# Routing logits of twelve token tiles: from matmuls on turned rows to products and sums on VectorE

## What is computed

```python
skip_score = x @ w_skip            # 512 numbers
do_compute = skip_score > 0
logits = xc @ w_gate               # 512 x 8
e_idx = np.argmax(logits, axis=1)
gate_w = softmax(logits)[e_idx]
out[do_compute] = xc + gate_w * (relu(xc @ w1[e]) @ w2[e])
```

## Time and profile before

| | us |
|---|---|
| median of 3 runs | 864.53 (864.14 to 866.72) |
| the profiled execution | 864.83 |
| its span, first to last instruction | 863.1 |
| attention and block 0, up to the first copy of x2 | 294.9 |
| blocks 1 to 4, told by the copies of x2 | 71.6 each |
| block 5 and the experts | 281.8 |

### The profile page before, as it was taken

How to read it: one execution, slowest core, us unless ns; L and a number is a source line. 1 busy time by engine, 2 the same in 40 slices (tenths; PEclk the granted TensorE clock), 3 DMA queues, 4 the chain that set the end, 5 groups by cost and what they waited for, 6 DMA issues and landing times.

```text
span 863.1 us, 15119 instructions
## 1 busy us (share of the span) xinstructions
PE 828.5 (96%) x4870; PEld 687.4 (80%) x4871; DVE 463.4 (54%) x1122; ACT 358.1 (41%) x870; POOL 228.9 (27%) x232
## 2 busy tenths in 40 slices
PE   5999999998799999999999999999998899999995
PEld 4777777775799998899898989989986677887884
DVE  4766676666533344435434444443665699375342
ACT  4766766674233322222232222222344387255241
POOL 3656655661444001001001001100011232222121
PEclk9999999999899999999999999999999999999998
DMA  6344444521425102021021010001142499455100
GB/s 145 96 110 120 122 117 109 156 68 54 148 62 179 73 19 92 1 83 27 3 74 28 10 73 1 25 1 74 55 129 102 146 322 343 163 173 182 31 26 8
DMA packets 97200, 80.93 MB, mean 94 GB/s; under 512 B 63420, under 2 KB 74940, under 8 KB 97152
## 3 DMA queue, kind: packets, MB, share of 16 engines
q1 hardware_dynamic: 94096, 75.31, 28.4%
q0 software_dynamic: 3056, 5.00, 1.8%
HBM read 65.18 MB, written 18.25 MB: 97 GB/s over the span
## 4 chain that ended last, share of the span: by engine, by line
PE 69%; DVE 2%; issue 1%; DVEq 1%; ACT 0%; POOL 0%; POOLq 0%; ACTq 0%
PE h_ps L1495 11%; PE out_ps L1495 11%; PE h_ps L1496 11%; PE h_ps L1497 11%; PE out_ps L1497 11%; PE out_ps L1496 11%; PE lg_ps L1546 2%; PE out_ps L1622 1%; PE tr_ps L1535 1%; PE tr_ps L1587 1%; DVEq L845 0%; DVE ht_lo L1261 0%; DVE xt_lo L1222 0%; DVE x2t L1251 0%; DVE tile_ids L1231 0%
## 5 line engine op out<-in xcount | busy, mean ns | idle before, releaser
L1352 ACT ACTIVATE ex<-h_ps 128x384 f32<-128x384 f32 x96 | 47.3, 493 | 295.5 <-PE h_ps L1497 295.5
L1191 DVE TENSOR_SCALAR ex<-ex 128x384 f32<-128x384 f32 x96 | 35.2, 366 | 229.8 <-ACT ex L1352 229.8
L1495 PE MATMUL h_ps<-xt_hi,wi_hi 128*128 128x384 f32 x384 | 134.0, 349 | 5.2 <-DVE xt_lo L1222 5.2
L1496 PE MATMUL h_ps<-xt_lo,wi_hi 128*128 128x384 f32 x384 | 130.7, 340 | 0.0
L1497 PE MATMUL h_ps<-xt_hi,wi_lo 128*128 128x384 f32 x384 | 130.6, 340 | 0.0
L1495 PE MATMUL out_ps<-wo_hi,gt 128*128 128x512 f32 x288 | 114.6, 398 | 0.0
L1497 PE MATMUL out_ps<-wo_hi,gt 128*128 128x512 f32 x288 | 113.9, 395 | 0.0
L1496 PE MATMUL out_ps<-wo_lo,gt 128*128 128x512 f32 x288 | 113.3, 393 | 0.0
L425 ACT ACTIVATE prob<-s_ps,negmax 128x128 f32<-128x128 f32 (+2 forms) x144 | 78.0, 549 | 13.5 <-DVE negmax L305 7.2
L1495 PEld LDWEIGHTS h_ps<-xt_hi,wi_hi 128*128 128x128 f32 x384 | 72.9, 190 | 8.5 <-DVE xt_lo L1222 5.8
L1496 PEld LDWEIGHTS h_ps<-xt_lo,wi_hi 128*128 128x128 f32 x384 | 73.0, 190 | 2.5
(11 more groups left out here) (171 smaller groups left out, 1673.5 us busy)
## 6 DMA issues: line engine op xcount, KB each, us to landing
w_raw<-in_moe_w_dram SPq DMA_DIRECT2D x56, 512.0 KB, 4.7
attn_t<-attn_sb SPq DMA_DIRECT2D x16, 288.0 KB, 2.2
x_raw<-attn_t SPq DMA_DIRECT2D x24, 192.0 KB, 2.8
out_dram<-x SPq DMA_DIRECT2D x18, 256.0 KB, 2.6
x_rows<-x SPq DMA_DIRECT2D x18, 256.0 KB, 2.8
raw_qk<-in_q_dram SPq DMA_DIRECT2D x32, 128.0 KB, 2.5
raw_qk<-in_k_dram SPq DMA_DIRECT2D x32, 128.0 KB, 2.5
v<-in_v_dram SPq DMA_DIRECT2D x32, 128.0 KB, 2.4
```

Of the source, the lines that this page charges most:

```text
L1191: dve.tensor_scalar(e, e, 1.0, -1.0, ALU.min, ALU.add).then_inc(em_done, 1)
L1352: act.activation(ex[:, f % 2], h_ps[:, f % 2, 0:NB], ACT.Exp).then_inc(ex_done, 1)
L1495: pe.matmul(dst, stat[0], mov[0], start=start, stop=False, skip_group_check=True)
L1496: pe.matmul(dst, stat[0], mov[1], start=False, stop=False, skip_group_check=True)
```

## The change

The logits of tiles 0 to 11 (DOTS is 12, the tiles of blocks 0 to 3) are made on VectorE, with `tensor_tensor_reduce`: product of the x2 row tile with one column of the gates, and its sum, for nine columns. The gates and the skip weights are broadcast from memory to all 128 partitions: `all_gates` lies in the memory of the raw w1 pieces, [128, 512, 8], so that one column is read with a step of eight floats, and `all_skip` in the memory of the fourth raw piece of w2. The products go to `dot_rows`, a bfloat16 scratch in the memory of x2t. For tile s of block b - 1 the nine instructions come in steps DOT_AT(s) to DOT_AT(s) + 3, as 3, 2, 2 and 2, with DOT_AT(s) = TR_AT(b, s), at the end of VectorE's part of the step; `choose` follows the last two in step RANK_AT - 1. `turn`, `x2t_copy` and `logits` remain for tiles 12 to 17. The loads of the first w1, and the fourth piece of the first w2, move behind the last of these instructions, at the end of block 4.

```diff
+    DOTS = TB * (LAST - 1)
+    DOT_AT = lambda s: RANK_AT(0, s) - 4
...
+        dot_rows = y.bitcast(BF16).rearrange("p (j d) -> p j d", j=2)
...
-        logit = sb("logit", [P, E + 1], F32)
+        all_gates = w1_raw[:, :, :, :].rearrange("p j o f -> p (j o f)").rearrange("p (d e) -> p d e", e=E)
+        all_skip = spare[:, 2, 0]
+        logits_sb = [sb(f"logit{j}", [P, E + 1], F32) for j in range(2)]
...
+            def broadcast_gates():
+                sp.dma_start(all_gates.rearrange("p d e -> p (d e)"),
+                             w_gate.rearrange("(o d) e -> o (d e)", o=1).broadcast_to([P, DM * E]))\
+                  .then_inc(all_gates_in, 16)
+                sp.dma_start(all_skip, w_skip.rearrange("(o d) -> o d", o=1).broadcast_to([P, DM]))\
+                  .then_inc(all_gates_in, 16)
...
-            for j in range(PIECES):
-                load_w1(sp, w1, 0, j, w1_raw, w1_in)
+            broadcast_gates()
...
-                    for j in (0, 1, 3):
+                    for j in (0, 1):
                         load_w2(0, j)
                 if b == LAST - 1:
                     sp.wait_ge(x_lo_done, KC * BLOCKS)
                     load_w2(0, 2)
+                    sp.wait_ge(route, (A_STEPS + B_STEPS) * DOTS)
+                    for j in range(PIECES):
+                        load_w1(sp, w1, 0, j, w1_raw, w1_in)
+                    load_w2(0, 3)
...
+            def dots(b, s, es):
+
+                t = TB * b + s
+                for e in es:
+                    if e == 0:
+                        dve.wait_ge(all_gates_in, 32)
+                        dve.wait_ge(x2_done, t + 1)
+                        wait(dve, probs_done, t - 1)
+                    wait(dve, dot_done, E * t + e - 1 if e > 1 else E * t)
+                    ins = dve.tensor_tensor_reduce(dot_rows[:, ((E + 1) * t + e) % 2], x2[s][:, :], all_skip if e == E else all_gates[:, :, e],
+                                                   1.0, 0.0, ALU.mult, ALU.add, logits_sb[t % 2][:, e:e + 1])
+                    ins.then_inc(route if e == E else dot_done, 1)
...
-                dve.wait_ge(lg_done, t + 1)
-                dve.wait_ge(const_done, 11)
+                logit = logits_sb[t % 2]
+                if t < DOTS:
+                    dve.wait_ge(const_done, 11)
+                else:
+                    dve.wait_ge(lg_done, t - DOTS + 1)
                 wait(dve, probs_done, t)
                 wait(dve, rk_done, t)
-
-                dve.tensor_copy(logit[:, :], lg_ps[:, 0:E + 1]).then_inc(route, 1)
+                if t < DOTS:
+                    dve.wait_ge(dot_done, E * (t + 1))
+                else:
+                    dve.tensor_copy(logit[:, :], lg_ps[:, 0:E + 1]).then_inc(route, 1)
...
                 for s in range(TB):
+                    if b and b < LAST and DOT_AT(s) <= f < DOT_AT(s) + 4:
+                        dots(b - 1, s, ((0, 1, 2), (3, 4), (5, 6), (7, 8))[f - DOT_AT(s)])
                     if b:
                         if f == RANK_AT(b, s) - 1:
                             choose(b - 1, s)
...
-                        act.wait_ge(tr_done, TB * (b - 1) + s + 1)
+                        t = TB * (b - 1) + s
+                        if t < DOTS:
+                            act.wait_ge(route, (A_STEPS + B_STEPS) * t + 1)
+                        else:
+                            act.wait_ge(tr_done, t - DOTS + 1)
...
-                        if f == TR_AT(b, s) + 1:
+                        if b == LAST and f == TR_AT(b, s) + 1:
                             x2t_copy(b - 1, s)
...
-                        if f == TR_AT(b, s):
+                        if b == LAST and f == TR_AT(b, s):
                             turn(b - 1, s)
-                        if f == TR_AT(b, s) + 2:
+                        if b == LAST and f == TR_AT(b, s) + 2:
                             logits(b - 1, s)
```

More of the change, by code:

```diff
@@ L773, in experts @@
         const_done = sem("f_const_done")
+        dot_done = sem("dot_done")
         gates_in = sem("gates_in")
+        all_gates_in = sem("all_gates_in")
         table_init = sem("table_init")
@@ L1370, in x2_copy @@
                         act.wait_ge(x2_out[s], 32 * b)
-                        act.wait_ge(tr_done, TB * (b - 1) + s + 1)
+                        t = TB * (b - 1) + s
[3 more added lines that the diff above has]
+                            act.wait_ge(tr_done, t - DOTS + 1)
                     act.activation(x2[s][:, :], out_ps[:, s, :], ACT.Copy).then_inc(x2_done, 1)
             def x2t_copy(b, s):
-                t = TB * b + s
-                act.wait_ge(tr_done, t + 1)
-                wait(act, lg_done, t)
+                u = TB * b + s - DOTS
+                act.wait_ge(tr_done, u + 1)
+                if u == 0:
+                    act.wait_ge(route, (A_STEPS + B_STEPS) * (DOTS - 1) + 1)
+                wait(act, lg_done, u)
                 act.activation(x2t[:, :, :], tr_ps[:, :].rearrange("p (k t) -> p k t", k=KC),
@@ L1384, in soften @@
                 act.wait_ge(route, (A_STEPS + B_STEPS) * t + A_STEPS)
-                act.activation(probs[:, :], logit[:, 0:E], ACT.Exp, bias=neg_top[:, :],
+                act.activation(probs[:, :], logits_sb[t % 2][:, 0:E], ACT.Exp, bias=neg_top[:, :],
                                accum_out=psum_row[:, :]).then_inc(probs_done, 1)
@@ L1532, in turn @@
                 pe.wait_ge(x2_done, t + 1)
-                wait(pe, x2t_done, t)
+                wait(pe, x2t_done, t - DOTS)
                 for k in range(KC):
@@ L1541, in logits @@
                 t = TB * b + s
-                pe.wait_ge(x2t_done, t + 1)
-                if t:
+                pe.wait_ge(x2t_done, t - DOTS + 1)
+                if t > DOTS:
                     pe.wait_ge(route, (A_STEPS + B_STEPS) * (t - 1) + 1)
@@ L1553, in ranks @@
                 pe.wait_ge(route, (A_STEPS + B_STEPS) * t + A_STEPS)
+                if t == 0:
+                    pe.wait_ge(const_done, 11)
                 if b == LAST:
```

## The result

| | before | changed |
|---|---|---|
| median, 10 runs each | 864.88 us (864.14 to 867.25) | 862.30 us (861.51 to 864.36) |
| ratio of the changed kernel to before | | 0.9969, 95% interval 0.9958 to 0.9979 |
| profiled execution, its span | 864.83, 863.1 | 863.67, 862.0 |

The change gains 2.6 us, 0.3%, where 15.2 us were forecast. The time lies in the range, but above 848 to 851, the forecast's own.

A forecast was written before the change was run, and what follows sets the result against it. TensorE was taken to bound blocks 1 to 4, VectorE having idle time; 9.5 us of logits and 5.7 of turns made 15.2, all else nothing: 864.83 - 15.2 = 849.6, or 849.3 us at the median. Range 847.5 to 868.

The forecast's parts named there:

- TensorE sheds 15.2 us: Blocks 1 to 4: twelve sets of logits (9.5 us) and twelve turns (5.7 us) leave TensorE, and that time is saved.
- A product costs 0.68 us: VectorE: one 512-element product and sum, built from neighbouring instructions, takes 0.68 us; low end 0.60, high end 1.24.
- rival A: VectorE, steps 3 to 14 of blocks 1 to 4: products take 1.24 us, TensorE waits; 866 to 882, near 874; chance 0.23.
- The port costs nothing: Products behind casts: up to four waits of 1.02 us a block for GpSimd's subtraction, hidden by VectorE's idle time.
- Room for 27 products, 27.2 us and 2.1 of lead: VectorE, steps 3 to 14: 50.5 us less 23.3 of other work leaves 27.2; the low half is 2.1 us early.
- The 23.3 us: VectorE's other work in steps 3 to 14: minimum, maximum, low half, casts, `choose`, `assign` and waits for the ranks.
- the tight places: Steps 7 and 11, three products after `assign`: VectorE 0.6 us late, covered by the lead; without it 4.8 us in all.
- The loads cost nothing: Broadcasts and moved w1 and w2 loads arrive in time: about 16 us spare, five loads taking about 10 of 34 us.

The follow-up runs named there:

- dense columns: Changed kernel with the gates first written column by column to a memory scratch, so a product reads consecutive floats: 849.86 us, ratio to before 0.9823.
- moved casts: Changed kernel with casts of x and GpSimd's subtractions moved to steps 0 to 2 in blocks 1 to 4, gates still strided: 850.06 us, ratio 0.9824.
- both together: Changed kernel with dense columns and moved casts at once: 849.34 us, ratio to before 0.9813.
- step of 16 bytes: Dense-column kernel with gates in groups of four columns (GK = 4): 856.72 us, ratio to before 0.9895.
- each product twice: Dense-column kernel with each product made twice, the first result unread: 879.03 us, ratio to before 1.0162.

## Why the prediction was wrong, point by point

- **TensorE sheds 15.2 us:** right. The three fitting variants have blocks of 67.7 us against 71.6, 15.6 us in four blocks. The dense columns, the moved casts and both together measure 15.7, 15.5 and 16.2 us less than the runs of before beside them (865.54).
- **A product costs 0.68 us:** this is the step that failed. It holds for one product in nine. The other eight read with a step of 32 bytes and took 1.18 us (1.10 from start to start). I had the case in hand (1.24 us, rival A), and chose the nearest row over it. That row read nothing with a step, so it said nothing on the question; nearness in size was no evidence. The Trainium skill's rule of 16-byte lines ("SBUF — State Buffer", section "Door 1") agrees with the jump between 8 and 16 bytes. It gives the penalty no size, so the 1.24 us that the prediction has "by either" does not follow from it. The other rule in the Trainium skill, of half rate for two non-bf16 sources ("Vector Engine (DVE) Microarchitecture Reference", section 7), does not show here: the dense product has two float32 sources and an accumulator, and takes 0.69 us. The page states the rule for one instruction shape; the trace calls the product CUSTOM_DVE_ANT_0, and whether it has that shape no run shows.
- **The port costs nothing:** right at 0.68 us, wrong at 1.18. Each of the four waits of a block is 0.83 us, not 1.02, and without them and the casts 1.18 us fits as well.
- **Room for 27 products, 27.2 us and 2.1 of lead:** right in the main, too kind near the edge. With the measured prices the demand is 23.3 + 24 x 1.10 + 3 x 0.61 + 4 x 0.83 = 54.9 us against 52.6, 2.3 over, where the blocks are 70.8 - 67.7 = 3.1 us longer; for the step of 16 bytes the same sum has 52.5, nothing over, and the blocks are 1.6 longer. Two terms are off. The 23.3 us still hold copies of the logits and waits for the ranks, which the changed kernel does not have. And the lead does not add 2.1 us to the room, as this table shows (us, means over the blocks, from the starts of VectorE's minimum; "most behind" is the most that a minimum starts behind the end of its exponential):

  | | step 3 to step 15 | step 15 to the next step 3 | most behind | TensorE waits for the low half |
  |---|---|---|---|---|
  | dense columns | 50.7 | 17.0 | 0.6 | no |
  | casts moved | 51.2 | 16.5 | 1.9 | no |
  | step of 16 bytes | 52.4 | 17.0 | 2.5 | yes |
  | the change | 54.2 | 16.5 | 2.7 | yes |
  | each product twice | 58.9 | 15.8 | 3.3 | yes |

  Of what steps 3 to 14 overrun, the rest of the block gives back 0.5 us in the changed kernel, nothing at 16 bytes and 1.2 with doubled products, never 2.1. The lead is real, since being 1.9 us behind costs nothing and 2.5 does, but it is used up right after the steps with three products. In the changed kernel the steps with two products behind them take VectorE 3.5 us, where TensorE needs 4.2, so it has caught up before the block ends, and the sum over twelve steps counts room that is no longer of use. With doubled products the two errors cancel (59.6 us in the sum against 58.9 in the trace, 2.1 of lead against 1.2), so the forecast of 74.7 us was met in part by luck. These are the tight places that the prediction named and priced at nothing.
- **Rival A, 866 to 882 us:** right in mechanism, too dark in size, since it took 1.24 us from start to start for all 27 products, where 24 took 1.10 and three 0.61. That is 33.5 - 28.2 = 5.3 us a block too much, and 0.2 us too much for each port wait. So the sign turned out positive: the block lost 3.1 of 3.9 us and kept 0.8.
- **The loads cost nothing:** right. In block 5 of the changed kernel every exponential and every split of w1 stands at the same distance from that block's copy of x2 as before, within 0.03 us.

## What to carry to other kernels

Before a tensor is laid out for a VectorE instruction, look at the byte step of its sources: a second source of float32 read with a step of 16 or 32 bytes made the product 1.6 to 1.7 times as long, one of 8 bytes was free, and eight small transfers that wrote the gates anew cost no time that shows. When work moves onto an engine with idle time, sum its demand over the steps that hold it, including waits for the port it shares, and ask how wrong a price may be before the room is gone. Here that was 1.01 us for each product, 0.86 with the port, and the one price that no row showed, 1.10 us, lay beyond it. Then look at the tightest steps by themselves: slack that comes after them does not help them.

## What was not expected of the hardware

- The product and sum of 128x512 float32 on VectorE takes the same time with the second source at steps of 4 and 8 bytes (0.69 us), 1.08 with 16 and 1.18 with 32.
- The port wait works in both directions: a VectorE product behind the first one is 0.83 us longer (1.18 to 2.0, dense 0.69 to 1.5), and GpSimd's subtraction goes from 1.02 to 1.90 us, as it waits for the product that had started. Once in sixteen GpSimd waited for both products (2.56 us), and the second was not stretched (0.73).
- TensorE's granted clock shortly after 219 us differed between executions of kernels that are the same up to there: 0.84, 0.77 and 0.81 in three profiles.
